# An attention and two-layer kernel on one core: the lone chunks' loads, scores and gates in another order

## The reference

```python
for t in range(S):
    m_new = np.maximum(f_gate[:, :, t] + m, i_gate[:, :, t])
    f_stab = np.exp(f_gate[:, :, t] + m - m_new)
    i_stab = np.exp(i_gate[:, :, t] - m_new)
    m = m_new
    C = f_stab[:, :, None, None] * C + i_stab[:, :, None, None] * np.einsum('bhd,bhe->bhde', vt, kt)
    n = f_stab[:, :, None] * n + i_stab[:, :, None] * kt
    h_tilde = np.einsum('bhde,bhe->bhd', C, qt)
    nq = np.einsum('bhd,bhd->bh', n, qt)[:, :, None]
    denom = np.maximum(np.abs(nq), 1.0)
    o = 1.0 / (1.0 + np.exp(-o_gate[:, :, t]))
    y[:, :, t] = o * h_tilde / denom
# x: y as [B * S, H * D]
x = (sigmoid(x @ w_gate) * (x @ w_val)) @ w_out
x = ((x @ w_a) * (x @ w_b)) @ w_out2
```

## Time and profile before

| what | value |
|---|---|
| median of 3 runs | 465.3 us |
| the runs | 465.39, 465.30, 464.38 us |
| the profiled execution | 464.92 us |
| its span, first to last instruction | 463.0 us |
| PE busy | 458.0 us, 99% of the span |
| DVE busy | 202.5 us, 44% |
| ACT busy | 195.4 us, 42% |
| POOL busy | 87.1 us, 19% |
| TensorE clock granted | 1.000 on average |

### The profile page before, as it was taken

How to read it: one execution, slowest core, us unless ns; L and a number is a source line. 1 busy time by engine, 2 the same in 40 slices (tenths; PEclk the granted TensorE clock), 3 DMA queues, 4 the chain that set the end, 5 groups by cost and what they waited for, 6 DMA issues and landing times.

```text
span 463.0 us, 6631 instructions
## 1 busy us (share of the span) xinstructions
PE 458.0 (99%) x2527; PEld 404.1 (87%) x2527; DVE 202.5 (44%) x363; ACT 195.4 (42%) x360; POOL 87.1 (19%) x99
## 2 busy tenths in 40 slices
PE   8999999999999999999999999999999999999997
PEld 6888899898989889888889889889988988998896
DVE  8877666766564644434132252222313122321313
ACT  5975838557392845234253352213212221311222
POOL 4484132312303020102454360000000000000000
PEclk9999999999999999999999999999999999999999
DMA  5788595453534460001322300000010000100001
GB/s 152 226 264 253 182 245 182 143 153 95 130 117 116 128 219 6 1 2 32 112 98 62 132 0 1 0 2 0 16 42 1 0 2 0 58 0 1 0 1 57
DMA packets 21449, 37.42 MB, mean 81 GB/s; under 512 B 2835, under 2 KB 15670, under 8 KB 21418
## 3 DMA queue, kind: packets, MB, share of 16 engines
q1 hardware_dynamic: 21050, 35.94, 25.4%
q10 hardware_dynamic: 208, 0.71, 0.4%
q0 software_dynamic: 160, 0.35, 0.2%
HBM read 34.91 MB, written 2.04 MB: 80 GB/s over the span
## 4 chain that ended last, share of the span: by engine, by line
PE 93%; DVE 2%; ACT 2%; issue 1%; DMA 1%; POOL 0%; DVEq 0%; POOLq 0%
PE bank L583 57%; PE bank L600 27%; PE bank L505 3%; PE bank L496 1%; PE bank L471 1%; ACT pt L690 1%; PE bank L519 1%; PE bank L561 1%; PE bank L531 1%; PE bank L480 1%; DMA f_row<-f_in 1%; DVE pt L896 0%; DVE s_row L860 0%; DVE m_row L877 0%; ACT L690 0%
## 5 line engine op out<-in xcount | busy, mean ns | idle before, releaser
L754 ACT CAST h_hi<-h_ff 128x512 fp32r<-128x512 f32 x72 | 44.6, 619 | 180.7 <-PE bank L600 95.2
L583 PE MATMUL bank<-xt,w_hi 128*128 128x512 f32 x360 | 118.6, 394 | 0.0
L971 DVE TENSOR_TENSOR h_lo<-h_ff,h_hi 128x512 fp32r<-128x512 f32 x72 | 52.8, 734 | 122.6 <-ACT h_hi L754 122.6
L965 DVE TENSOR_TENSOR h_ff<-bank,s_ff 128x512 f32<-128x512 f32 x72 | 49.7, 691 | 102.1 <-PE bank L583 98.1
L583 PE MATMUL bank<-xt,w_lo 128*128 128x512 f32 x216 | 84.3, 390 | 0.0
L583 PEld LDWEIGHTS bank<-xt,w_hi 128*128 128x128 f32 x360 | 65.8, 188 | 12.6 <-DVE t_st L933 0.4
L747 ACT ACTIVATE s_ff<-bank 128x512 f32<-128x512 f32 x72 | 43.0, 598 | 72.3 <-PE bank L583 71.8
L583 PE MATMUL bank<-xt,w_hi_end 128*128 128x512 f32 x180 | 58.9, 392 | 0.0
L583 PE MATMUL bank<-xt,w_hi_mid 128*128 128x512 f32 x180 | 58.9, 392 | 0.0
L583 PEld LDWEIGHTS bank<-xt,w_lo 128*128 128x128 f32 x216 | 40.5, 188 | 8.7
L600 PE MATMUL bank<-w_hi,h_hi 128*128 128x320 f32 x144 | 45.0, 312 | 0.0
(11 more groups left out here) (128 smaller groups left out, 676.5 us busy)
## 6 DMA issues: line engine op xcount, KB each, us to landing
w_raw<-w_in SPq DMA_DIRECT2D x24, 544.0 KB, 4.1
vk<-vk_in SPq DMA_DIRECT2D x12, 344.0 KB, 3.5
levels<-a_scratch SPq DMA_DIRECT2D x7, 512.0 KB
k_both<-kq_in SPq DMA_DIRECT2D x18, 120.0 KB
q_blk<-kq_in SPq DMA_DIRECT2D x18, 120.0 KB
y<-rows_t SPq DMA_DIRECT2D x12, 160.0 KB, 1.9
q<-kq_in SPq DMA_DIRECT2D x10, 180.0 KB
osig_b<-o_in SPq DMA_DIRECT2D x8, 160.0 KB, 3.0
```

The lines of the kernel that those rows point to most:

```text
L583: mm = pe.matmul(up_bank(u, gv)[:, :], w_part(low, f, (gv * 3 + kt) * P, P), xt[:, xb * TOK + g * TG:xb * TOK + (g + 1) * TG], start=(j == ...
L754: act.copy(h_hi[u % 2][:, :], h_ff[u % 2][:, :]).then_inc(act_h, 1)
L965: dve.tensor_tensor(h_ff[u % 2][:, :], up_bank(u, 1)[:, :], s_ff[u % 2][:, :], ALU.mult).then_inc(dve_h, 1)
L971: dve.tensor_tensor(h_lo[u % 2][:, :], h_ff[u % 2][:, :], h_hi[u % 2][:, :].bitcast(F32), ALU.subtract).then_inc(dve_hlo, 1)
```

## The change

It changes the order of the prologue on each engine, in six places:

- The memset of chunk 0's query tile is cut into three by blocks of heads (`BLOCKS`), and each of its three query DMAs waits for its own; they stand ahead of `load_k(1)` on SP now.
- PE does `scores(0, 1)` right behind `scores(0, 0)`. `spread(1)` comes between the two scores of chunk 1.
- `values(0)` is cut in two halves of four heads (`values_of`), with `spread(2)` between them. The memset of the fix is cut in two for chunk 0, so that each half has its own.
- On SP, `load_q(2)` stands ahead of `load_rows(2)`, and `load_v(1)` moves behind both. `load_rows(3)` moves ahead of `load_scaled(2)`.
- On ACT, the load of the output gates moves behind `weigh(1, 1)`.
- The decay rows of chunks 2 to 5 move from before the output gates' Sigmoid to behind `gate_cols(2)`, ahead of `x_high(0)`.

The diff:

```diff
--- before.py
+++ after.py
@@ -269,6 +269,8 @@
             return XY[1] if g == 0 else XY[tb % 2]
 
 
+        BLOCKS = ((0, 3), (1, 3), (2, 2))
+
         @block.sync
         def _(sp):
             def load_rows(n):
@@ -296,7 +298,9 @@
                 s = set_of(n)
                 if n >= BATCH:
                     load_k(n)
-                for j, k in ((0, 3), (1, 3), (2, 2)):
+                for j, k in BLOCKS:
+                    if n == 0:
+                        sp.wait_ge(dve_zero, j + 1)
                     own = slice(j * HD, (j + 1) * HD)
                     sp.dma_start(q_blk[s][own, 3 * j * P:(3 * j + k) * P],
                                  kq3_in[n, own, 3 * P:(3 + k) * P]).then_inc(ld_q[s], 16)
@@ -352,9 +356,8 @@
 
             sp.dma_start(f_row[:, :], f_in).then_inc(ld_gate, 16)
             load_k(0)
+            load_q(0)
             load_k(1)
-            sp.wait_ge(dve_zero, 1)
-            load_q(0)
             sp.dma_start(ident[:, :], consts_in[:, 0:P]).then_inc(ld_ident, 16)
             sp.wait_ge(act_zero, 1)
             load_q(1)
@@ -364,16 +367,16 @@
             sp.wait_ge(tri_set1, 1)
             load_rows(1)
             load_v(0)
-            load_v(1)
+            load_q(2)
             sp.wait_ge(dve_split, 4)
             load_rows(2)
-            load_q(2)
+            load_v(1)
             sp.wait_ge(act_irow, 1)
             store_rows(f_row, i_dram, 1, 2, st_irow)
-            sp.wait_ge(dve_zero, 3)
+            load_rows(3)
+            sp.wait_ge(dve_zero, 5)
             sp.wait_ge(st_irow, 16)
             load_scaled(2)
-            load_rows(3)
             sp.wait_ge(dve_dec, 1)
             sp.dma_start(d_dram, d_row[:, :]).then_inc(st_dec, 16)
             load_v(2)
@@ -480,6 +483,16 @@
                     mm = pe.matmul(st[:, at:at + k * P], k3[s][:, x * P:(x + 1) * P], own, start=True, stop=True)
                 mm.then_inc(pe_s, 1)
 
+            def values_of(n, half):
+
+                pe.wait_ge(dve_fix, half + 1)
+                pe.wait_ge(ld_v[n], 16)
+                for h in range(half * HEADS // 2, (half + 1) * HEADS // 2):
+                    mm = pe.matmul(value_bank(n)[:, h * VW:(h + 1) * VW], pt[n][:, h * P:(h + 1) * P],
+                                   vk[n][:, h * VW:(h + 1) * VW], start=(h == 0), stop=(h == HEADS - 1))
+                if half:
+                    mm.then_inc(pe_fv, 1)
+
             def values(n):
 
                 s, p = set_of(n), n % 2
@@ -497,7 +510,7 @@
                                        cst[p][:, h * VW:(h + k) * VW], start=(x == 0), stop=False)
                     mm.then_inc(pe_f, 1)
                 if n <= ALONE:
-                    pe.wait_ge(dve_fix, n + 1)
+                    pe.wait_ge(dve_fix, n + 2)
                 else:
                     pe.wait_ge(dve_p, 2 * n + 2)
                 pe.wait_ge(ld_v[s], 16 * (use_of(n) + 1))
@@ -607,6 +620,7 @@
             pe.wait_ge(dve_warm, 1)
             turn_over(9)
             scores(0, 0)
+            scores(0, 1)
             pe.wait_ge(ld_ident, 16)
             columns(0, 0, dve_gate, 5)
             columns(0, 1, dve_rows, 1)
@@ -615,12 +629,12 @@
             pe.wait_ge(act_cols, 2)
             columns(1, 0, dve_gate, 9)
             columns(1, 1, dve_rows, 2)
-            scores(0, 1)
             scores(1, 0)
+            spread(1)
             scores(1, 1)
-            spread(1)
+            values_of(0, 0)
             spread(2)
-            values(0)
+            values_of(0, 1)
             to_state(0)
             scores(2, 0)
             scores(2, 1)
@@ -789,18 +803,18 @@
             gate_cols(1)
             weigh(0, 1)
             weigh(1, 0)
+            weigh(1, 1)
             act.dma_start(osig_a[:, :], o_in[:, 0:ALONE * DM]).then_inc(ld_oa, 16)
-            weigh(1, 1)
             act.wait_ge(act_cols, 3)
             weigh(2, 0)
             weigh(2, 1)
-            for c in range(2, CHUNKS):
-                i_rows(c)
             act.wait_ge(ld_oa, 16)
             act.activation(osig_a[:, :], osig_a[:, :], ACT.Sigmoid).then_inc(act_o, 1)
             weigh(3, 0)
             weigh(3, 1)
             gate_cols(2)
+            for c in range(2, CHUNKS):
+                i_rows(c)
             x_high(0)
             x_high(1)
             w_high(0)
@@ -894,9 +908,10 @@
                 dve.wait_ge(pe_s, 2 * n + half + 1)
                 own = slice(half * HALF, (half + 1) * HALF)
                 dve.tensor_tensor(pt[s][:, own], score_bank(n, half)[:, :], pt[s][:, own], ALU.mult).then_inc(dve_p, 1)
-                if half and n <= ALONE:
-                    dve.wait_ge(dve_p, 2 * n + 2)
-                    dve.memset(pt[s][LO:LO + 1, LO - 1::P], 0.0).then_inc(dve_fix, 1)
+                if n == 0 or half and n <= ALONE:
+                    dve.wait_ge(dve_p, 2 * n + half + 1)
+                    of = own if n == 0 else slice(0, 2 * HALF)
+                    dve.memset(pt[s][LO:LO + 1, of.start + LO - 1:of.stop:P], 0.0).then_inc(dve_fix, 1)
 
             def combine(n):
 
@@ -993,7 +1008,8 @@
 
 
             dve.memset(h_hi[0][:, 0:P].bitcast(F32), 0.0).then_inc(dve_warm, 1)
-            dve.memset(q_blk[0][:, :], 0.0).then_inc(dve_zero, 1)
+            for j, k in BLOCKS:
+                dve.memset(q_blk[0][:, 3 * j * P:(3 * j + k) * P], 0.0).then_inc(dve_zero, 1)
             dve.memset(rst[:, 0:2 * P], 1.0).then_inc(dve_gate, 1)
             dve.wait_ge(dve_gate, 1)
             dve.memset(by3(rst, 0, 2)[:, :, 0], 0.0).then_inc(dve_gate, 1)
```

## The result

| | median of 6 | from | to |
|---|---|---|---|
| before | 465.35 us | 464.38 | 2612.65 |
| changed | 473.41 us | 470.94 | 478.85 |

The account below looks back on a forecast made before the run. It took PE as the bound, with the time set by when the first `up` starts. +2.07 us at scores(3,0) less 0.4 of cover gave +1.65 on the 465.3 median: 466.9 us, range 465.2 to 468.4.

Parts of the forecast that it names:

- What bounds the kernel: PE is busy 99%; the first `up` start, 32.81, sets the time, and delay there comes out one for one.
- First queries by thirds, scores(0,1) ahead: Start of the prologue: scores(0,0) start at about 5.3, m_prev loses its overlap with POOL; gain 0.3 us.
- The queue of SP, and POOL behind it: Late load_v(1) delays POOL's v_w and chunk 3's queries; PE stands 2.4 us, scores(3,0) start 2.07 us later.
- What is given back behind it: From scores(3,0) to the first `up`: existing wait and slack absorb 0.4 us, no new wait, 1.65 us late arrives.
- the clock: Rival: after PE's 2.4 us stand, a lower clock slows scores(3) and small work, +1.7 us on top, 468.6; chance 0.05.
- Shared DMA engines: Rival: load_v(1) lands 0.7 us later beside the output gates' load; +2.3, 467.6 us; chance 0.17.

Follow-up runs that it names:

- experiment 1: The changed kernel with load_v(1) put back right behind load_v(0) on SP; 466.62 us, ratio 1.0035.
- experiment 2: The changed kernel with POOL issuing chunk 3's k and query loads ahead of weigh_v(1), load_v(1) still late; 468.28 us, ratio 1.0025.
- experiment 10: The changed kernel with load_v(1) back behind load_v(0) and PE waiting ahead of scores(3,0) for POOL's second x_n; 472.50 us, ratio 1.0085.
- 13: The changed kernel, load_v(1) back, PE waiting for POOL's second x_n ahead of scores(3,0), ten 512-column matmuls behind scores(3,1); 472.36 us, ratio 1.0112.
- 14: hold_x_narrow: the changed kernel, load_v(1) back, PE waiting for POOL's second x_n ahead of scores(3,0), 20 42-column matmuls behind scores(3,1); 477.86 us.
- 4: after_fillers: the changed kernel with twelve 512-column matmuls of zeros on PE ahead of scores(3,0); 473.55 us, ratio 1.0048.
- 3: The kernel before with load_v(1) moved behind load_rows(2) and load_q(2) on SP; 469.87 us, ratio 1.0071.
- 7: v1_back_pool_first: the changed kernel with load_v(1) back behind load_v(0) and POOL's chunk 3 loads ahead of weigh_v(1); 469.11 us, ratio 1.0043.
- 9: The changed kernel with load_v(1) back behind load_v(0) and PE waiting ahead of scores(3,0) until POOL scaled chunk 2's q; 467.46 us, ratio 1.0022.
- 11: The changed kernel with load_v(1) behind load_q(2), ahead of the dve_split wait and load_rows(2); 470.14 us, ratio 1.0058.
- 12: The changed kernel with ten 512-column matmuls of zeros behind scores(3,1); 473.85 us, ratio 1.0137.

## Why the forecast was wrong

- *What bounds the kernel.* Right: the stretch behind the first `up` is unchanged, and what was late there was late at the end (8.97 us at the loop, 8.7 in the span).
- *First queries by thirds, scores(0,1) ahead.* Right in the trace that it comes sooner: the scores start at 5.12 (forecast 5.3), the m_prev steps take 0.15 us. The size was off, with 0.3 us forecast: spread(3), the last work ahead of scores(3,0), starts at 18.06 in place of 19.05, 1.0 us sooner. All of it was lost in the stand, as the forecast had it. In experiment 1's profile, without the stand, only 0.13 us of it is there at scores(3,0), and PE waits 0.70 us for `x_raw` ahead of columns(2). I had no row for that.
- *The queue of SP, and POOL behind it.* Right in every link and nearly in size: `load_v(1)` at 10.24 (forecast 11.0), `v_w` at 13.42 (14.4), the scores of chunk 3 at 21.50 (21.7), the stand 2.72 us (2.4). The last query load went out at 16.7 and landed 4.8 us later (4.0 taken), which made up for the earlier issue. Experiments 1 and 2 each take away one link, and the stand goes.
- *What is given back behind it.* Right that no new wait came: neither turn(1) nor scores(4,0) stands. The store of the decay rows went out at 26.84 (forecast 25.7). But PE ran at half speed there, which can hide a wait. In experiment 2's profile, at full clock and without the stand, turn(1) waits 0.63 us for `x_low(0)`; the forecast's 0.2 us of margin was thin.
- *The step that failed: the clock.* The sum priced PE's wait by its length alone, and put what the clock does behind it at nothing. It stood among the rivals at 0.05, at +1.7 us for scores(3) and "the small work behind them". By the mean clocks it was the case in all six executions of the changed kernel, and in the profiled one it cost 7.10 us (20.28 us for 13.18). The mistake in size was to let the low level end soon after the scores. It lasted until 39.6, over values(2), values(3) and three of the four turns. (The +1.7 doesn't follow from its own words either: 0.6 us for each of two scores and "as much again" are 2.4.) The mistake in the chance was to take a gap of 0.37 us, behind which the clock went up, as evidence on one of 2.4. Experiment 10 shows that a stand of this length is enough by itself. Experiments 13 and 14 show, by their mean clocks, that wide matmuls behind it shorten the low level and narrow ones don't. The Trainium skill ("TensorE: Matmul & The Clock Gate", section "HAM oscillation — how this bites in real kernels") warns of waits for DMA behind which the array is back at half rate, and I had cited it and given it one chance in twenty. This case's trace agrees on the fall, but its wait, 2.72 us, is shorter than those of the page's example.
- *Shared DMA engines.* Not seen as priced: `load_v(1)` landed at 13.35, 3.1 us after its issue, faster than the 3.3 taken. But landing times differ between executions: the same load, issued at 10.29, held POOL until 15.36 in the fillers' profile, with the same order ahead of it. So one profile doesn't rule the rival out.
- *The range.* It ended at 468.4, below all six executions. A range that took in the rival at its right size would have had to reach 474, and the two executions beyond that, 476.3 and 478.9, were low for longer still, by their clocks. The forecast also said that a measurement tells 0.2% from no change; the intervals of the runs here are 0.2 to 0.6% to either side.

What stays open: why some executions of the kernel before lose clock too (10 of the 35 beside the first four experiments had a mean clock of 0.996 or less), and what decides between a short and a long spell at the low level, which is the difference between 469 and 476 us in experiment 10. The profiles show eleven spells: 17.1 us in the changed kernel, 20.5 in experiments 3 and 10, some 13.6 in 7 and 14, 6.8 in 9, 11 and 13, 3.4 in 4, 12 and the first of 14. Each ended while scores or wide matmuls ran, or less than half a microsecond behind them. But scores(3) ended it in experiments 4 and 12 and not in 10, so the width of the work isn't all of it.

## What to carry to other kernels

Price a new wait of TensorE twice: once for its length, and once for the clock behind it, by what follows, and as a span and not as one number. A stand of 2.7 us in front of 20 us of mostly narrow matmuls cost 7 us more than itself in the profiled execution, and less or more in others; with ten wide matmuls behind such a stand no execution fell under a mean clock of 0.989, but their own time took the gain. And before a load goes back in a queue, follow not the tile but everything that is queued behind whoever waits for it: here it was one `v` tile that was there for POOL at 10.65 and that TensorE needed only for values(1) at 16.56, and POOL's queue also carried chunk 3's queries.

## What the runs showed of the hardware

- The granted clock went to 0.50 at 22.5, behind a stand of 2.72 us, and stayed there until 39.6 us, with PE at 5.00 of 5.00 us busy. Behind stands of 0.96 and 1.46 us it stayed at 1.00; in two other profiles it fell behind one of 1.59 (v1_back_pool_first) and one of 1.67 (hold_x_narrow).
- How long it stays low differs with the same instructions behind it: 3.4 us in after_fillers, 17.1 in the changed kernel.
- It also fell without a gap right ahead of it: in hold_x_narrow at 29.2 us, after 5 us of unbroken work, most of it narrow, behind a stand of 2.03 us.
- At the low level sixteen records of value matmuls take 3.55 us (1.92 at the high one), a spread 1.20 (0.71).
- The same load of 344 KB, in the same place of the same order, was there for POOL at 13.42 in one profile and at 15.36 in another.
